# Expert gates carried inside the gathered token rows, in a one-core attention, MLP and top-1 MoE kernel

## The reference, cut to what matters

```python
logits = x @ w_gate                                  # [N, 8]
expert_idx = np.argmax(logits, axis=1)
logits_shift = logits - logits.max(-1, keepdims=True)
probs = np.exp(logits_shift)
probs /= probs.sum(-1, keepdims=True) + 1e-09
gate_w = probs[np.arange(N), expert_idx]
for e in range(E):
    mask = expert_idx == e
    xe = x[mask]
    h = np.maximum(xe @ w1[e], 0.0)
    out[mask] = gate_w[mask, None] * (h @ w2[e])
```

## Time and profile before

| | us |
|---|---|
| median of 3 runs (lowest, highest) | 604.36 (604.26, 604.59) |
| span of the profiled execution | 604.2 |
| PE busy | 561.4 (93%) |
| DVE busy | 324.1 (54%) |
| ACT busy | 225.4 (37%) |
| POOL busy | 106.6 (18%) |

### The profile page before, as it was taken

How to read it: one execution, slowest core, us unless ns; L and a number is a source line. 1 busy time by engine, 2 the same in 40 slices (tenths; PEclk the granted TensorE clock), 3 DMA queues, 4 the chain that set the end, 5 groups by cost and what they waited for, 6 DMA issues and landing times. The chain is left out here.

```text
span 604.2 us, 9045 instructions
## 1 busy us (share of the span) xinstructions
PE 561.4 (93%) x3322; PEld 479.0 (79%) x3322; DVE 324.1 (54%) x529; ACT 225.4 (37%) x349; POOL 106.6 (18%) x139
## 2 busy tenths in 40 slices
PE   5888899999999999999999999659999999999991
PEld 4777788888877888887888887459999999998991
DVE  7556644455455554446456665326665665666510
ACT  1112333233352433226334554225455554554410
POOL 6666400000000000000000010240324224134101
PEclk9999899999999999999999999959999999999996
DMA  7666433332233232332232545444656657463000
GB/s 279 210 209 201 154 114 105 104 98 75 90 106 121 77 132 104 104 104 68 106 139 100 186 152 208 80 112 149 239 172 243 212 185 260 176 223 125 23 1 33
DMA packets 20492, 84.30 MB, mean 140 GB/s; under 512 B 5100, under 2 KB 5100, under 8 KB 16880
## 3 DMA queue, kind: packets, MB, share of 16 engines
q1 hardware_dynamic: 15088, 71.34, 34.4%
q0 software_dynamic: 4224, 10.50, 6.1%
q10 hardware_dynamic: 1152, 2.10, 0.9%
HBM read 78.67 MB, written 7.35 MB: 142 GB/s over the span
## 5 line engine op out<-in xcount | busy, mean ns | idle before, releaser
L856 DVE TENSOR_TENSOR ewl<-stage,ewh 128x1024 fp32r<-128x1024 f32 x64 | 78.1, 1224 | 23.4 <-ACT ewh L724 22.9
L544 PE MATMUL bank<-xh,gvh 128*128 (+1 forms) x288 | 77.3, 391 | 0.0
L544 PE MATMUL bank<-xh,gvl 128*128 (+1 forms) x288 | 77.0, 390 | 0.0
L544 PE MATMUL bank<-xl,gvh 128*128 (+1 forms) x288 | 77.0, 389 | 0.0
L944 DVE TENSOR_TENSOR sig<-bank,sig 128x512 f32<-128x512 f32 x36 | 24.9, 692 | 85.3 <-ACT sig L760 85.3
L724 ACT ACTIVATE ewh<-stage 128x1024 fp32r<-128x1024 f32 x64 | 67.0, 1052 | 1.6 <-DMA stage<-expert_w 1.6
L544 PEld LDWEIGHTS bank<-xh,gvh 128*128 128x128 f32 x288 | 54.2, 189 | 11.4 <-issue 0.3
L544 PEld LDWEIGHTS bank<-xl,gvh 128*128 128x128 f32 x288 | 54.1, 188 | 11.2
L544 PEld LDWEIGHTS bank<-xh,gvl 128*128 128x128 f32 x288 | 54.1, 188 | 11.2
L822 ACT ACTIVATE ehh<-bank 128x256 fp32r<-128x256 f32 x64 | 24.6, 384 | 93.5 <-PE bank L676 92.9
L922 DVE TENSOR_TENSOR gvl<-stage,gvh 128x1024 fp32r<-128x1024 f32 x36 | 44.6, 1239 | 26.2 <-ACT woh L724 26.1
(11 more groups left out here) (134 smaller groups left out, 886.8 us busy)
## 6 DMA issues: line engine op xcount, KB each, us to landing
stage<-expert_w SPq DMA_DIRECT2D x28, 1024.0 KB, 5.0
stage<-mlp_w SPq DMA_DIRECT2D x36, 768.0 KB, 4.3
stage<-attn_in SPq DMA_DIRECT2D x24, 512.0 KB, 4.7
stage<-expert_w POOLq DMA_DIRECT2D x8, 512.0 KB, 5.7
x_rows<-x ACTq DMA_DIRECT2D x8, 256.0 KB, 3.3
x_rows<-x SPq DMA_DIRECT2D x4, 256.0 KB, 2.3
out<-ys,idx_now POOLq DMA_INDIRECT x16, 4.0
gx<-x_rows,idx_now POOLq DMA_INDIRECT x14, 3.5
```

The costliest lines, as they stand in the source:

```text
L544: last = mm(bank[:, where, :], wt[:, k, :], (xh, xl)[x][:, k, bass.ds(g * GT, GT)], start=(at == 0), stop=(at == 3 * KD - 1))
L856: V.tensor_tensor(dst, src, high.bitcast(F32), ALU.subtract).then_inc(inc, 1)
```

## The change

The rows in HBM become 520 numbers (2080 bytes) instead of 512: 512 features and the 8 shifted logits. DVE's step 3 writes the shifted logits straight into the last 8 columns of `x2`, now one tile of 4 x 520. Stores of rows wait for that step, and ACT's stores move from f = 2, 3, 4, 5 to f = 3, 4, 5, 5. `gate_rows`, its store, its wait, all 16 gate gathers and the exponential over all tokens go. Each expert's `tokens` gets two small exponentials on ACT (one for each `gx`) and three small instructions on DVE, which make the gates of that expert's tokens. The load into `stage3` now waits until PE has transposed the first expert's rows (`gx_read` 4).

```diff
+ROW = DM + E
-        x2_rows = nc.dram_tensor("x2_rows", [N, DM], F32, kind="Internal").ap()
-        gate_rows = nc.dram_tensor("gate_rows", [N, 1], F32, kind="Internal").ap()
+        x2_rows = nc.dram_tensor("x2_rows", [N, ROW], F32, kind="Internal").ap()
-        gate_now = [sb(f"gate_now{i}", [P, 1]) for i in range(4)]
+        gate_now = [sb(f"gate_now{i}", [P, 2]) for i in range(2)]
-        x2 = [sb(f"x2_{i}", [P, DM], F32, region2) for i in range(GTT)]
+        x2 = sb("x2", [P, GTT, ROW], F32, region2)
-        gx = [sb(f"gx{i}", [P, DM], F32, region2) for i in range(2)]
+        gx = [sb(f"gx{i}", [P, ROW], F32, region2) for i in range(2)]
+        expo = sb("expo", [P, 2, E], F32, region2)
+        den, den_eps = [sb(f"den{i}", [P, 2], F32, region2) for i in range(2)]
...
+            sp.wait_ge(route, (NG - 1) * STEPS + 3)
             for t in range(GTT):
                 sp.wait_ge(rows_ready, (NG - 1) * GTT + t + 1)
                 sp.dma_start(x2_rows[(NG - 1) * GT + t * P:(NG - 1) * GT + (t + 1) * P, :],
-                             x2[t][:, :]).then_inc(x2_stored[t], 16)
-            sp.wait_ge(gate_ready_all, 1)
-            sp.dma_start(gate_rows.rearrange("(t p) o -> p (t o)", p=P), gate[:, :],
-                         allow_slow_non_contiguous=True).then_inc(gates_stored, 16)
-            sp.wait_ge(gates_stored, 16)
+                             x2[:, t, :]).then_inc(x2_stored[t], 16)
             sp.wait_ge(slots_ready, 1)
+            sp.wait_ge(gx_read, 4)
             sp.dma_start(stage[3][:, :], expert_w[1, 3]).then_inc(landed[3], 16)
...
             def gather(x, par):
                 pool.wait_ge(gx_read, x * 2 + 2)
+                pool.wait_ge(expo_ready, x)
                 copy_idx(x, par)
                 pool.wait_ge(idx_ready, 1)
                 pool.wait_ge(now_ready, x * 2 + 2)
                 for i in range(2):
                     fetch(gx[i], x2_rows, idx_now[2 * par + i][:, 0:1], gx_landed[i])
-                for i in range(2):
-                    fetch(gate_now[2 * par + i], gate_rows, idx_now[2 * par + i][:, 0:1], gate_landed[i])
             def first_gather():
-                pool.wait_ge(gate_clear, 4)
                 pool.wait_ge(gx_read, 2)
                 pool.wait_ge(idx_ready, 1)
                 for i in range(2):
                     fetch(gx[i], x2_rows, idx[:, i:i + 1], gx_landed[i])
                 copy_idx(0, 0)
-                pool.wait_ge(gates_stored, 16)
-                for i in range(2):
-                    fetch(gate_now[i], gate_rows, idx[:, i:i + 1], gate_landed[i])
...
             def store_rows(fin, t):
                 act.wait_ge(rows_ready, fin * GTT + t + 1)
-                act.dma_start(x2_rows[bass.ds(fin * GT + t * P, P), :], x2[t][:, :]).then_inc(x2_stored[t], 16)
+                act.wait_ge(route, fin * STEPS + 3)
+                act.dma_start(x2_rows[bass.ds(fin * GT + t * P, P), :], x2[:, t, :]).then_inc(x2_stored[t], 16)
...
                         if f >= 2:
                             rows_out(fin, f - 2, ROWS_BANK)
-                            store_rows(fin, f - 2)
+                        for t in ((), (), (), (0,), (1,), (2, 3))[f]:
+                            store_rows(fin, t)
...
-            act.wait_ge(route, (NG - 1) * STEPS + 3)
-            nc.scalar.activation(expo[:, :, :], spread[:, :, :], ACT.Exp).then_inc(exp_ready, 1)
...
+                act.wait_ge(den_step, x * 2)
+                for i in range(2):
+                    last = nc.scalar.activation(expo[:, i, :], gx[i][:, DM:], ACT.Exp)
+                last.then_inc(expo_ready, 1)
...
-                act.wait_ge(gate_landed[0], x * 16 + 16)
+                act.wait_ge(gate_ready_x, x + 1)
                 act.wait_ge(y_stored[0], x * 16)
                 nc.scalar.activation(ys[0][:, :], bank[:, Y_BANK, 0:DM], ACT.Copy,
-                                     scale=gate_now[2 * par][:, 0:1]).then_inc(y_act, 1)
+                                     scale=gate_now[par][:, 0:1]).then_inc(y_act, 1)
...
             def choose(fin):
-                now = spread[:, bass.ds(fin * GTT, GTT), :]
+                now = x2[:, :, DM:]
                 dve.wait_ge(logits_psum, fin + 1)
+                for t in range(GTT):
+                    dve.wait_ge(x2_stored[t], fin * 16)
...
-            dve.wait_ge(exp_ready, 1)
-            after(V.tensor_reduce(den[:, :], expo[:, :, :], AX_X, ALU.add))
-            after(V.tensor_scalar(den_eps[:, :], den[:, :], 1e-9, None, ALU.add))
-            V.reciprocal(gate[:, :], den_eps[:, :]).then_inc(gate_ready_all, 1)
...
+                dve.wait_ge(expo_ready, x + 1)
+                V.tensor_reduce(den[:, :], expo[:, :, :], AX_X, ALU.add).then_inc(den_step, 1)
+                dve.wait_ge(den_step, x * 2 + 1)
+                V.tensor_scalar(den_eps[:, :], den[:, :], 1e-9, None, ALU.add).then_inc(den_step, 1)
+                dve.wait_ge(den_step, x * 2 + 2)
+                V.reciprocal(gate_now[par][:, :], den_eps[:, :]).then_inc(gate_ready_x, 1)
...
-                dve.wait_ge(gate_landed[1], x * 16 + 16)
+                dve.wait_ge(gate_ready_x, x + 1)
```

More of the change, by code:

```diff
@@ L95, in bass_linear_attention_mlp_moe @@
         token_at = sb("token_at", [P, NT, NCOLS], F16, region0)
-        spread = sb("spread", [P, NT, E], F32, region0)
-        expo = sb("expo", [P, NT, E], F32, region0)
         ohb = sb("ohb", [P, GTT, E], BF16, region0)
@@ L104, in bass_linear_attention_mlp_moe @@
         ri = [sb(f"ri{i}", [P, GTT], I32, region0) for i in range(4)]
-        den, den_eps, gate = [sb(f"gate_step{i}", [P, NT], F32, region0) for i in range(3)]
         most = sb("most", [P, 1], F32, region0)
@@ L215, in bass_linear_attention_mlp_moe @@
         table_psum = sem("table_psum")
-        exp_ready = sem("exp_ready")
         here_ready = sem("here_ready")
@@ L219, in bass_linear_attention_mlp_moe @@
         tail = sem("tail")
-        gate_ready_all = sem("gate_ready_all")
-        gates_stored = sem("gates_stored")
         idx_ready = sem("idx_ready")
@@ L224, in bass_linear_attention_mlp_moe @@
         now_ready = sem("now_ready")
-        gate_clear = sem("gate_clear")
-        gate_landed = [sem(f"gate_landed{i}") for i in range(2)]
+        expo_ready = sem("expo_ready")
+        den_step = sem("den_step")
+        gate_ready_x = sem("gate_ready_x")
         gx_read = sem("gx_read")
@@ L404, in _ @@
                 nc.gpsimd.memset(gx[i][:, :], 0.0).then_inc(gx_read, 1)
-            for i in range(4):
-                nc.gpsimd.memset(gate_now[i][:, :], 0.0).then_inc(gate_clear, 1)
             for t in range(GTT):
@@ L467, in experts @@
                         pool.wait_ge(y_act, x + 1)
-                        nc.gpsimd.tensor_tensor(gate_now[0][:, :], gate_now[0][:, :], iota_row[:, 0:1], ALU.mult)
+                        nc.gpsimd.tensor_tensor(score[:, 0:1], score[:, 0:1], iota_row[:, 0:1], ALU.mult)
                     if par == 0:
@@ L779, in rows_out @@
                 act.wait_ge(x2_stored[t], fin * 16)
-                copy(x2[t][:, :], bank[:, where, :]).then_inc(rows_ready, 1)
+                copy(x2[:, t, 0:DM], bank[:, where, :]).then_inc(rows_ready, 1)
             def store_rows(fin, t):
                 act.wait_ge(rows_ready, fin * GTT + t + 1)
-                act.dma_start(x2_rows[bass.ds(fin * GT + t * P, P), :], x2[t][:, :]).then_inc(x2_stored[t], 16)
+                act.wait_ge(route, fin * STEPS + 3)
+                act.dma_start(x2_rows[bass.ds(fin * GT + t * P, P), :], x2[:, t, :]).then_inc(x2_stored[t], 16)
             def first_half(g, fin=None):
@@ L1093, in expert @@
                 dve.wait_ge(y_psum, x * 2 + 2)
-                dve.wait_ge(gate_landed[1], x * 16 + 16)
+                dve.wait_ge(gate_ready_x, x + 1)
                 dve.wait_ge(y_stored[1], x * 16)
-                V.tensor_scalar(ys[1][:, :], bank[:, Y_BANK + 1, 0:DM], gate_now[2 * par + 1][:, 0:1], None,
+                V.tensor_scalar(ys[1][:, :], bank[:, Y_BANK + 1, 0:DM], gate_now[par][:, 1:2], None,
                                 ALU.mult).then_inc(y_dve, 1)
```

## The result

The changed kernel takes **589.33 us** (median of 4 runs, 589.17 to 591.97), beside 604.48 for the kernel before (median of 4, 604.26 to 606.29). The ratio is 0.9752 with an interval of 0.9722 to 0.9783, so it is faster by 15 us. The forecast was 592.9 with a range from 590.8 to 597.5: the sign and the main cause held, and the gain was larger than the range allowed, by 1.5 us.

What follows compares the result with a forecast made beforehand. PE was taken as the bound in the experts, idling 10.17 us before them for row gathers held up by the gates' small store. 604.2 - 9.73 - 2.07 + 0.35 = 592.75, forecast 592.9 us, range 590.8 to 597.5.

Steps and rivals of the forecast that it cites:

- the small store and the wait for rows: Before the first expert: without the gates' store, first row gathers run like later ones; first product starts 9.73 us earlier.
- the seam: Between the MLP and the experts, at two thirds of the span: PE idles 10.17 us, waiting for the first rows.
- Rival A: First row gather is slow by itself, not through the store of gates: 604.7 us, no change; chance 6%.
- rival B: First gather lands about 3 us later than forecast and the clock falls as well: 598.0 us; chance 8%.
- rows of 2080 bytes cost next to nothing: Row gathers, first expert and experts 2 to 7: longer rows cost 0.05 us at seven places, a loss of 0.35.
- C: Last 32 bytes of each row go as separate pieces, up to 2.0 us at seven gathers: 606.6 us; chance 3%.
- D: Longer rows moderately dearer by the page's rule, 0.5 us at each of seven gathers: 596.1 us; chance 12%.
- the small costs of nothing: ACT's exponentials and table load, DVE's three instructions, moved stores, POOL's queue and the delayed load: each costed at 0.
- E: ACT reloads its table at each expert, 1.283 us at f = 5: at most 8.4 more, 601.3 us; chance 3%.
- POOL's wait for the exponentials: Gather for expert 1 waits for expert 0's exponentials until 392.8, still there by 399.1 when PE wants it; cost 0.
- from there to the end each expert takes as long as before: After the first outward product, every expert's time stays unchanged but for tenths at the gathers.
- the clock, 2.07: First expert: clock stays full, first matmul to first outward product takes 2.88 instead of 4.95; if it falls, 0.

Runs made afterwards that it cites:

- the second execution of the kernel before: The kernel before, run again with no edit as a yardstick: 604.30 us, ratio 0.9999, span 600.6.
- after_rel0: Changed kernel plus an unused tile of 1856 bytes per partition ahead of `exh`, token tiles back at the weights' offset modulo 2048: 591.93 us.

## Why the prediction was right or wrong

**Right: the small store and the wait for rows.** I forecast 9.73 for the earlier first product, and it was 10.01, of which 0.23 lies ahead of the seam (the fillers began at 383.42, not 383.65). Against the second execution of the kernel before it was 8.42, so that the number agrees to 0.3 is in part luck. The rows came at 388.34 and 389.44, forecast 388.33 and 389.71. The cause is shown both ways, by putting the store back (+9.8) and by changing its form in the kernel before. Rival A falls, and so does the late gather of rival B. B's other half, a clock that falls, came true. The reading that the DMA engines "were not crowded" was wrong: it took one stretch for ten.

**Right: rows of 2080 bytes cost next to nothing.** Both medians are 3.5, and the later experts' gathers show no dearer wait: PE's weight loads wait at most 0.22 us for them, where one waited 0.18 before. So C and D fall. The Trainium skill (DMA: Bandwidth & Descriptors, How a descriptor splits into AXI transactions) would have had more at each gather; the 3.5 us on both sides don't show it. I also worked its rule out too high: if the table begins on such a boundary, every row begins on a multiple of 32 bytes and takes 9 transactions, never 10. So an estimate by that page of the Trainium skill is an eighth more, some 0.4 us a gather, instead of a quarter. Only ACT's stores of such rows grew, and those lie under matmuls: 5.1 us to landing in the row shown above, 3.3 before. What that growth comes from wasn't tried; two of the stores are also issued together now.

**Right: the small costs of nothing.** The table was loaded once for the exponentials, at 390.75, 1.28 long, partly under PE's first product (from 391.59), so E falls. The cushions shrank. ACT and DVE, timelines of expert 0 at the places of the earlier trace rows:

```profile
410.81 0.39 ACT L814 ACTIVATE ehh<-bank 128x256 fp32r<-128x256 f32 x1 [0.26 <-PE bank L664]
```
```profile
411.75 0.16 DVE L1072 TENSOR_REDUCE den<-expo 128x2 f32<-128x16 f32 x1
...
413.99 0.42 DVE L1081 SCALAR_TENSOR_TENSOR ehl<-bank,ehh 128x256 fp32r<-128x256 f32 x1 [0.18 <-ACT ehh L814]
```

ACT's idle time ahead of its Relu copy went from 0.52 to 0.26, so the exponentials took less of it than the 0.46 that I counted. DVE's ahead of the low part at f = 7 went from 0.65 to 0.18. Both are above zero, and PE has no idle time there. They are also close to zero, so there is little room for more such instructions. POOL's wait for the exponentials ended with its index copies at 392.58, forecast 392.8.

**Wrong: "from there to the end each expert takes as long as before".** This sentence failed, and it carried the miss. The changed tile sizes moved the operands of PE's matmuls, and a step went from 2.82 to 2.76 us. By medians that is 2.6 (591.93 against 589.33). The 16 gathers of gates that POOL no longer issues shortened its closing drain by 1.3; the sum had no term for it. The trace of before has the step of 2.82 and the drain of 4.71, but nothing in it says that this change would move either.

**Mis-sized: the clock, 2.07.** "I take full clock" rested on idle pieces of at most 1.5 us. The clock fell in 391 to 392, and the term measured 0.62, no more than the same kernel varies by. With fillers it is there (2.92 us to the first outward product). The case in which it falls was priced, at 0, and with it alone the forecast would have been 2.1 later, further from what was measured: this miss hid part of the other.

**Misread: the base.** I set the forecast 0.15 above a span. An execution's time lies 1.7 above its span, so that profiled execution took some 605.9 by the 1.7 of the other runs, 1.5 above the median. The forecast itself is not touched by it, since the same gains taken from the median of 604.36 give 592.9 too. But the 1.1 of chance on POOL stood in the rows that I worked from, and in no term of the sum.

The sum of spans closes. Against the forecast span of 592.75, the measured 587.5 is 5.25 lower: 6.07 for experts and tail, 0.35 for rows that cost nothing, 0.28 for the first product, less 1.45 for the clock. By medians, of the 15.1 us the small store has 9.8 and placement 2.6, and the drain's row gives 1.3, together 13.7; the remaining 1.4 is within the scatter of medians between comparisons (603.2 to 605.3 for the kernel before). With the tiles put back the change takes 591.93, which would have been within the range. That the sign and the seam came out is the mechanism; that the total lay only 3.6 off is in part luck, since an over-counted clock stood against gains that had no term.

## What to carry to other kernels

When a gather that an engine waits for takes longer than its like, list what was issued beside it: 6 KB in pieces of 4 bytes cost more here than 1 MB did. Read the DMA share over the whole wait, since one stretch of 1 us can mislead. A change in tile sizes can alter the pace of matmuls that it doesn't touch, so compare their start-to-start times before explaining a difference by the edit itself. Where POOL issues DMAs, look at its closing drain too, which was 1.3 us longer here with 16 more of them.

## What was unexpected of the hardware

- 1536 pieces of 4 bytes on one queue held two gathers of another queue from 3.5 to 12.5 us. The DMA engines were busy 0.64 on average meanwhile and moved at most 61 GB/s; 1 MB beside the gathers held them to 5.4.
- POOL's closing drain took 3.41 us with 40 DMAs issued and 4.71 with 56, though 16 of them had landed long before: 0.08 us each on average.
- Placement of operands moves the pace of PE by 2% either way: steps of 2.81 to 2.82 at distances 0, 64 and 1024, and 2.76 at 192, where in the MLP 192 costs 7.7 us.
- PE's clock fell although no idle time was longer than 1.50 us (0.55, 0.47 and 1.50), with only transposes in between.
- POOL took about 1 us longer over the same two copies behind its loop in some executions and not in others, in the kernel before (1.31 and 0.30).
- The stretch from the first expert's first product to its first outward product varied between executions by up to 1 us, with the same instructions in it (4.33 in the changed kernel, 5.29 in `after_rel0`).
